# Attention and two MoE layers on one core: four raw weight buffers in the first tile, and the attention's group loop re-ordered

## The reference

```python
# attention: 8 batches x 8 heads, S = 576, D = 64, 32 memory slots
a   = softmax(phi)                          # (b, h, s, 32)
k_m = einsum('bhsm,bhsd->bhmd', a, k)       # and v_m alike
attn = softmax(q @ k_m.T / sqrt(64))        # over the 32 slots
x = (attn @ v_m)  -> (4608 tokens, 512)
# first MoE: one dense layer
h = x @ w_in                                # 512 -> 2048
x = (h * sigmoid(1.702 * h)) @ w_out        # 2048 -> 512
# second MoE: 8 experts, top 1
e = argmax(x @ w_gate); w = softmax(x @ w_gate)[e]
out = w * sigmoid(x @ w_output_gate)[e] * (relu(x @ w1[e]) @ w2[e])
```

## Time and profile before

| | us |
|---|---|
| median of 3 runs | 1346.61 (1345.87 to 1348.1) |
| the profiled execution | 1348.39 |
| its span | 1346.8 |
| PE busy | 1309.3 (97%) |
| PEld busy | 1054.9 (78%) |
| DVE busy | 634.2 (47%) |
| POOL busy | 554.6 (41%) |
| ACT busy | 388.6 (29%) |
| mean granted clock of TensorE | 0.994 |

### The profile page before, as it was taken

The page is one execution under the profiler, slowest core; times in us unless marked ns, Lnnn a source line. Parts: engine busy times, 40 slices in busy tenths (PEclk is TensorE's granted clock), DMA queues, the critical chain, the costliest instruction groups (busy, mean ns, idle before and its releaser), DMA issues.

```text
span 1346.8 us, 23538 instructions
## 1 busy us (share of the span) xinstructions
PE 1309.3 (97%) x6866; PEld 1054.9 (78%) x6867; DVE 634.2 (47%) x1291; ACT 388.6 (29%) x725; POOL 554.6 (41%) x648
## 2 busy tenths in 40 slices
PE   5997999999999999999999999999999999999997
PEld 3455888888888888888888888887788888888886
DVE  4893243443533434334334343447555555555553
ACT  3672222222222322222222222223322222222221
POOL 2455764454434442443444334512443242433332
PEclk9998999999999999999999999999999999999999
DMA  9996357555565464654654546557874778549872
GB/s 362 401 423 233 103 179 204 200 195 173 200 185 188 168 195 156 186 188 164 178 191 168 189 164 177 185 175 234 255 206 99 224 236 257 161 135 266 238 241 63
DMA packets 152924, 274.26 MB, mean 204 GB/s; under 512 B 16947, under 2 KB 54084, under 8 KB 150308
## 3 DMA queue, kind: packets, MB, share of 16 engines
q1 hardware_dynamic: 96100, 204.30, 43.6%
q10 hardware_dynamic: 43584, 37.37, 11.4%
q0 software_dynamic: 13184, 31.88, 7.4%
HBM read 144.98 MB, written 100.45 MB: 182 GB/s over the span
## 4 chain that ended last, share of the span: by engine, by line
PE 90%; DMA 4%; DVE 2%; issue 1%; POOL 1%; SPq 1%; ACT 0%; ACTq 0%; POOLq 0%
PE ps L699 29%; PE ps L733 28%; PE ps L774 15%; PE ps L803 15%; DMA phT<-in_phi 3%; PE ps L743 1%; DMA raw<-in_moe_w_out 1%; DMA raw<-in_moe_w_in 1%; DVE sc L1150 0%; DVE scs L1152 0%; DVE scs L1161 0%; PE ps L618 0%; PE ps L671 0%; POOL W L1541 0%; DMA cq<-ch 0%
## 5 line engine op out<-in xcount | busy, mean ns | idle before, releaser
L699 PE MATMUL ps<-xs,W 128*128 (+1 forms) x1728 | 420.1, 392 | 5.1 <-POOL W L1541 5.1
L733 PE MATMUL ps<-W,gs 128*128 128x512 f32 x1728 | 415.4, 389 | 1.2 <-POOL W L1531 1.1
L699 PEld LDWEIGHTS ps<-xs,W 128*128 128x128 f32 x1728 | 324.5, 189 | 75.2 <-issue 8.2
L733 PEld LDWEIGHTS ps<-W,gs 128*128 128x128 f32 x1728 | 324.5, 188 | 69.4 <-issue 1.5
L1225 DVE TENSOR_TENSOR gate<-ps,gate 128x512 f32<-128x512 f32 x144 | 99.5, 691 | 373.5 <-ACT gate L969 373.1
L969 ACT ACTIVATE gate<-ps 128x512 f32<-128x512 f32 x144 | 86.1, 598 | 474.9 <-PE ps L699 459.6
L803 PE MATMUL ps<-W,chT 128*128 (+1 forms) x936 | 218.2, 389 | 1.0 <-DVE chT L1362 0.8
L774 PE MATMUL ps<-W,cx 128*128 (+1 forms) x936 | 218.5, 389 | 0.5 <-issue 0.5
L1595 POOL CAST whi<-raw 128x512 fp32r<-128x512 f32 x128 | 83.6, 653 | 317.2 <-DMA raw<-in_moe_w 317.2
L803 PEld LDWEIGHTS ps<-W,chT 128*128 128x128 f32 x936 | 175.6, 188 | 38.1 <-issue 1.8
L774 PEld LDWEIGHTS ps<-W,cx 128*128 128x128 f32 x936 | 175.6, 188 | 37.4 <-issue 1.1
(11 more groups left out here) (163 smaller groups left out, 781.3 us busy)
## 6 DMA issues: line engine op xcount, KB each, us to landing
W<-expert_scratch SPq DMA_DIRECT2D x24, 2048.0 KB, 10.3
raw<-in_moe_w SPq DMA_DIRECT2D x128, 256.0 KB
expert_scratch<-whi SPq DMA_DIRECT2D x128, 256.0 KB, 2.6
expert_scratch<-raw SPq DMA_DIRECT2D x128, 256.0 KB, 2.8
cq<-ch ACTq DMA_DIRECT2D x156, 128.0 KB
kvm<-in_kv SPq DMA_DIRECT2D x16, 1152.0 KB, 10.6
crec<-record_scratch POOLq DMA_DIRECT2D x160, 64.0 KB
qT<-in_q SPq DMA_DIRECT2D x16, 576.0 KB, 8.6
```

The lines of the kernel that those rows point to most:

```text
L699: mm = pe.matmul(ps[:, f % 2, :], W[:, col:col + P], xs[:, bass.ds(x0 + (x_lo * K1 + c) * T, T)], start=(c == 0 and w_lo + x_lo == 0), sto ...
L733: mm = pe.matmul(ps[:, 2 + s, :], gs[:, f % 2, g_lo, s * P:(s + 1) * P], w_out_sb[:, f, w_lo, :], start=(f == 0 and g_lo + w_lo == 0), sto ...
```

## The change

Four edits.

1. Two more raw buffers (`raw2`), used in turn with the old ones from chunk 4 on; `load_w(n)` waits for the split of chunk n-4, and chunks 6 and 7 for the k/v product of group 14, since raw2 overlies kv buffer 2. Chunks 4 to 7 are issued before the store of batches 0 to 4, and the four half stores of batches 5 and 6 between the loads of chunks 8 to 11. The quarters of w_in are loaded at groups 4, 5, 9 and 10, and split by GpSimd one group later.
2. ScalarE's list: the scaled k/v product first, k's copy ahead of the exp of the scores, a's copy behind it, and the exp of phi of group g+2 (was g+1). SP loads phi two groups ahead.
3. The scores' maximum is subtracted by GpSimd (last group: by VectorE) ahead of normalize(g-2). VectorE's list is scores_max(g-1), inverses(g-2), phi's maximum of g+2, transpose of g-2. The last group's normalization has a semaphore of its own, and VectorE does both last `inverses` in a row.
4. The k/v product goes to columns 384 to 511 of bank 6, a scores' bank; it waits until VectorE has transposed that bank's half of the scores of g-1, and no longer for an output copy. mm1(0,1) stands ahead of both halves of group 14, and x_out of group 14 is between the sigmoid and the cast of step 0.

```diff
-        QUARTER = (5, 6, 9, 10)
+        QUARTER = (4, 5, 9, 10)
+        w_raw = [raw[:, 0, :], raw[:, 1, :], raw2[:, 0, :], raw2[:, 1, :]]
+        def w_slot(n):
+            return n % 2 if n < K1 else n % 4
...
             def load_w(n, src):
-                wait(sp, s_wlo, n - 1)
-                sp.dma_start(raw[:, n % 2, :], src).then_inc(s_wraw[n % 2], 16)
+                if n in (K1 + 2, K1 + 3):
+                    sp.wait_ge(s_kv, NG - 1)
+                else:
+                    wait(sp, s_wlo, n - 1 if n < K1 + 2 else n - 3)
+                sp.dma_start(w_raw[w_slot(n)], src).then_inc(s_wraw[w_slot(n)], 16)
...
-            load_kv(0)
-            load_q(0)
-            for g in range(1, NG):
-                load_phi(g)
+            load_phi(1)
+            for g in range(NG):
                 load_kv(g)
                 load_q(g)
+                if g + 2 < NG:
+                    load_phi(g + 2)
...
-            load_w(K1, w_out_v[0])
-            load_w(K1 + 1, w_in_part(0, 1))
+            for c in range(2):
+                load_w(K1 + 2 * c, w_out_v[c])
+                load_w(K1 + 2 * c + 1, w_in_part(c, 1))
             store_kept(0, FIRST, s_xfirst)
-            for b in range(FIRST, KEPT):
-                store_kept(b, 1, s_xkept)
...
-                            if f:
+                            if f >= 2:
                                 load_w(K1 + 2 * f, w_out_v[f])
+                                if f < 4:
+                                    store_kept(FIRST + f - 2, 1, s_xkept, (0,))
                                 load_w(K1 + 2 * f + 1, w_in_part(c, k))
+                                if f < 4:
+                                    store_kept(FIRST + f - 2, 1, s_xkept, (1,))
...
-                wait(pe, s_xo, 2 * (g - 4) + 1)
+                wait(pe, s_dv, DVE_A * (g - 1) + 1)
                 pe.wait_ge(s_am, g + 1)
-                out_of = lambda h: ps[h * M:(h + 1) * M, 4, 3 * P:4 * P].rearrange("p (w d) -> p w d", w=2)
+                out_of = lambda h: ps[h * M:(h + 1) * M, 6, 3 * P:4 * P].rearrange("p (w d) -> p w d", w=2)
...
             mm1(0, 0)
             out_half(NG - 3, 1)
+            mm1(0, 1)
             out_half(NG - 2, 0)
-            mm1(0, 1)
             out_half(NG - 2, 1)
...
# ScalarE
             def group(g):
                 u = g % 2
-                if g + 1 < NG:
-                    exp_phi(g + 1, 1 - u)
+                kv_scale(g, u)
                 if g >= 4:
                     x_out(g - 4, 1)
-                if g >= NG - 2:
-                    for c in range(2):
-                        first_x_hi(2 * (g - (NG - 2)) + c)
-                kv_scale(g, u)
+                if g == NG - 1:
+                    first_x_hi(2)
+                k_out(g)
                 if g:
                     exp_scores(g - 1, 1 - u)
-                k_out(g)
                 if g + 1 < NG:
                     a_out(g + 1)
+                if g + 2 < NG:
+                    exp_phi(g + 2)
+                elif g == NG - 2:
+                    first_x_hi(0)
+                    first_x_hi(1)
+                else:
+                    first_x_hi(3)
                 if g >= 3:
                     x_out(g - 3, 0)
...
# VectorE
             def group(g):
-                u = g % 2
-                if g + 1 < NG:
-                    phi_in(g + 1)
-                inverses(g, u, g >= 2, True)
-                if g:
-                    less_max(g - 1, 1 - u)
+                scores_max(g - 1, (g - 1) % 2)
+                inverses(g - 2 if g >= 2 else None, g + 1 if g + 1 < NG else None)
+                if g + 2 < NG:
+                    phi_in(g + 2)
                 if g >= 2:
                     attn_out(g - 2)
...
+            scores_max(NG - 1, 1)
+            dve.wait_ge(s_dv, DVE_A * NG)
+            dve.tensor_tensor(by_m(1), by_m(1), each_m(1, 0), ALU.subtract).then_inc(s_mx, 1)
             dve.wait_ge(b_xhi, K1)
             dve.tensor_tensor(xs[:, (2 * K1 - 1) * T:2 * K1 * T], kept(K1 - 1), xs[:, (K1 - 1) * T:K1 * T].bitcast(F32),
                               ALU.subtract).then_inc(s_x3, 1)
-            inverses(NG, 0, True, False)
-            less_max(NG - 1, 1)
+            inverses(NG - 2)
+            inverses(NG - 1)
+            dve.wait_ge(s_rin, NG + 3)
+            dve.tensor_tensor(by_m(1), by_m(1), each_m(1, 2), ALU.mult).then_inc(s_x15, 1)
             attn_out(NG - 2)
...
# GpSimd
+            def less_max(g, u):
+                pool.wait_ge(s_dv, DVE_A * (g + 1))
+                by_m = sc[u][:].rearrange("p (n m) -> p n m", m=M)
+                pool.tensor_tensor(by_m, by_m, scs[:, u, 0:1, 0:SB].rearrange("p o n -> p n o").broadcast_to([P, SB, M]),
+                                   ALU.subtract).then_inc(s_mx, 1)
             for g in range(NG):
+                if g == NG - 1:
+                    first_x_lo(0)
+                if g:
+                    less_max(g - 1, 1 - g % 2)
                 if g >= 2:
                     normalize(g - 2, g % 2)
                 v_blocks(g, g % 4)
...
-                if g == NG - 2:
-                    for c in range(2):
-                        first_x_lo(c)
+            first_x_lo(1)
             first_x_lo(2)
             normalize(NG - 2, 0)
```

More of the change, by code:

```diff
@@ L159, in build @@
             kvs = sbt(a, "kvs", [P, 2 * D])
-            kv2 = sbt(a, "kvm2", [P, QA * D * 2])
+            with ExitStack() as a2:
+                kv2 = sbt(a2, "kvm2", [P, QA * D * 2])
+            sbt(a, "before_raw2", [P, 6 * T - 2 * S - P - 2 * D])
+            raw2 = sbt(a, "raw2", [P, 2, CH])
             pT.append(sbt(a, "pT1", [P, S]))
             sbt(a, "to_512_third", [P, 64])
[L163 to L167, removed]
+            q2 = sbt(a, "qT2", [P, QA // 2, HG, M])
+            ph2 = sbt(a, "phT2", [P, S])
             qT, kvm, phT = [q0, q1, q2], [kv0, kv1, kv2], [ph0, ph1, ph2]
@@ L268, in build @@
                                                         (nc.sync, "sync_waits_passed"), (nc.tensor, "pe_waits_passed"), (nc.scalar, "act_waits_passed"))}
-        s_wraw = [sem(f"w_raw_loaded{u}") for u in range(2)]
+        s_wraw = [sem(f"w_raw_loaded{u}") for u in range(4)]
         s_whi = sem("w_hi")
@@ L452, in load_q, with store_kept @@
                 sp.dma_start(qT[g % 3][:].rearrange("p c h n -> p (c h n)"), q[g * P:(g + 1) * P, :]).then_inc(s_q[g % 3], 16)
-            def store_kept(b, n, stored):
+            def store_kept(b, n, stored, us=range(2)):
                 sp.wait_ge(s_xo, 4 * (b + n))
-                for u in range(2):
+                for u in us:
                     sp.dma_start(xT_dram[2 * u * P:(2 * u + 2) * P, b * S:(b + n) * S].rearrange("(a p) n -> p a n", a=2),
@@ L1069, in act_tile @@
                         x_hi(t + 1, f - 11)
[L1071 to L1074, removed]
+            g_sigmoid(0, 0)
+            for i in range(2):
+                x_out(NG - 2, i)
+            g_hi(0, 0)
+            for i in range(2):
+                x_out(NG - 1, i, (6, 4)[i])
             store_last()
@@ L1137, in phi_in @@
                 dve.wait_ge(s_phi[g % 3], 16 * (g // 3 + 1))
+                wait(dve, s_aT, g - 1)
                 dve.tensor_reduce(amax[:, g % 2, 0:1], phT[g % 3][:], AX.X, ALU.max, negate=True).then_inc(s_amax, 1)
@@ L1152, in less_max, with inverses, attn_out @@
                 dve.tensor_reduce(scs[:, u, 0, 0:SB], by_m(u), AX.X, ALU.max).then_inc(s_dv, 1)
[L1153 to L1160, removed]
+            def inverses(scores=None, phi=None):
+                u = scores % 2 if scores is not None else 1 - phi % 2
+                n = scores + 4 if scores is not None else phi + 1
+                lo, hi = (0 if scores is not None else SB), (SB + 1 if phi is not None else SB)
+                if scores is not None:
+                    dve.wait_ge(s_ex, scores + 1)
                     dve.tensor_reduce(scs[:, u, 1, 0:SB], by_m(u), AX.X, ALU.add).then_inc(s_sm, 1)
-                    wait(dve, s_sm, g - 1)
-                if phi:
-                    wait(dve, s_aT, g + 1)
+                    dve.wait_ge(s_sm, scores + 1)
+                if phi is not None:
+                    dve.wait_ge(s_aT, phi + 1)
                 dve.tensor_scalar(scs[:, u, 1, lo:hi], scs[:, u, 1, lo:hi], 1e-9, None, ALU.add).then_inc(s_eps, 1)
-                wait(dve, s_eps, g + 1)
+                dve.wait_ge(s_eps, n)
                 dve.reciprocal(scs[:, u, 2, lo:hi], scs[:, u, 1, lo:hi]).then_inc(s_rin, 1)
-            def attn_out(g):
-                wait(dve, s_nrm, g + 1)
+            def attn_out(g, by_pool=True):
+                if by_pool:
+                    dve.wait_ge(s_nrm, g + 1)
                 wait(dve, s_o, 2 * (g - 1))
@@ L1194, in _ @@
             phi_in(0)
+            phi_in(1)
+            dve.wait_ge(s_cst, 2 * 16)
+            inverses(phi=0)
+            inverses(phi=1)
             wait(dve, s_cst2, 6 * 16)
@@ L1206, in _ @@
```

(18 more changed lines are left out.)

60 lines of the change are left out of this document (35 added, 25 removed).

## The result

The median is 1341.43 us in 17 executions (1338.01 to 1346.16), before 1346.74 in 17 (1345.82 to 1349.06). The ratio is 0.9963, 95% interval 0.995 to 0.9975: 5.0 us faster, 3.4 to 6.7. The forecast was 6.5. The spread is the news: it has grown from 3.2 to 8.2 us, with seven executions from 1338.0 to 1340.6 (the short ones), six from 1345.7 to 1346.2 (the long ones), and only four between, among them the median. The profiled one is among the long ones: 1346.1, span 1344.5.

The account below looks back on a forecast made before the run. TensorE's matmul stream was taken to bound the kernel from its last hole, before mm1(0,4). That stream's start moves from 131.9 to 125.4 (9.3 from buffers, less the tail): 6.5 us faster, median 1340.1, range 1335.0 to 1344.5.

Parts of the forecast that it names:

- the hole in mm1(0,0): Attention's tail: TensorE idles 3.1 us before mm1(0,0)'s last quarter, waiting for GpSimd's increment of b_xlo behind normalize(14).
- the low clock behind it: Tail: the 3.1 us idle brings TensorE's lower clock, costing 2.0 us (ends 0 and 2.7) before mm1(0,2).
- Part 1: First MoE tile's weights: four buffers end the split stalls, 13.75 us from mm1(0,2) to mm1(0,4); alone worth 9.3 us.
- Part 2's loop: VectorE's attention loop per group, now 4.88 us: becomes 5.26 with eps held, 4.81 if not held.
- eps is held: VectorE's addition of eps is blocked in every group until GpSimd's new subtraction ends, 0.4 us after the sums.
- rival E: Attention loop: GpSimd's two tensor_tensors stretched from 1.16 to 1.6 us, loop 6.14; 6.3 us slower, 1352.9; chance 0.08.
- The start: Attention's first groups: phi(1) loaded first brings VectorE's first scores to 17.4 us from 20.03, 2.6 earlier.
- The step that failed: Attention on TensorE: k's copy ahead of exp and the product's wait for transposes cost nothing, covered by the output halves.
- The tail: Last scores to mm1(0,2): from 96.7 to 109.7, then 2.0 more for the clock, 111.7; what was won is given back.
- B: Clock stays up through the tail's hole (8.5 us faster), eps unheld (9.4), or both (11.4); about 1337.2; chance 0.28.
- D: TensorE's idle only moves to waits for b_xlo and kept stores, mm1(0,4) near 130; about 1346; chance 0.07.
- C: Weights stay late: chunk 11 lands 12 us after issue, mm1(0,4) at 127.4; 4.5 us faster, 1342.1; chance 0.10.

Follow-up runs that it names:

- e2: Kernel before with the four raw buffers and their load and store order alone, attention as before: median 1339.94 us, ratio 0.9944.
- e7: e5 with VectorE's inverses(g-2) ahead of scores_max(g-1) and GpSimd's normalize(g-2) ahead of the maximum's subtraction: median 1345.92 us, ratio 0.9985 to the kernel before.
- e5: Changed kernel with 8 filler matmuls ahead of the scores and 10 behind them in groups 0 to 2: median 1339.19 us, ratio 0.9938 to the kernel before.
- e9: Changed kernel with the k/v product back in bank 4, waiting for group g-4's output copy: median 1340.45 us in 5 executions, ratio 0.9945 to the kernel before.
- e12: e9's kernel run once more, product back in bank 4: median 1339.81 us in 6 executions, ratio 0.9944 to the kernel before.
- e1: Changed kernel run again without an edit: median 1339.96 us (1338.65 to 1347.07, 9 executions), ratio 0.9955 to the kernel before.
- e3: Changed kernel with two raw buffers and the old store and load order, leaving the attention's edits alone: median 1348.29 us, ratio 1.0004 to the kernel before.
- e6: e5 without the addition of 1e-9 (eps) to the attention's sums: median 1335.80 us, ratio 0.9912 to the kernel before.
- e8: e7 with GpSimd's count of x's part 3 in b_xlo ahead of normalize(14): median 1345.69 us, ratio 0.9983 to the kernel before.
- e10: e6 with GpSimd's count of x's part 3 in b_xlo ahead of normalize(14): median 1335.54 us, ratio 0.9907 to the kernel before.
- e4: Changed kernel with 32 filler matmuls ahead of the first transposes and 40 behind them: median 1343.18 us, ratio 0.9964 to the kernel before.

## Why the prediction was right, and where it was off

The sign, the range and the size (5.0 of 6.5) held, but the size by luck: two errors of opposite sign met in a median that stands between two groups of executions. mm1(0,4), forecast at 125.4 and within 123 to 126, was at 128.45 in the long execution (start +6.2, tail -3.2) and at 121.73 in the short one (-0.5 and -3.2). The last scores, forecast at 96 to 97.5, were in the range in the short one alone, and the hole in mm1(0,0) and the low clock behind it were not as forecast in either.

*Part 1* was right to 0.1 us: e2's mm1(0,4) at 122.59, predicted 122.6; 13.73 from mm1(0,2) in the changed kernel, predicted 13.75; and the splits kept 2.3 us ahead, 2.8 in e2. A split did wait for its load before mm1(0,4), 0.44 us in the long execution, 0.95 in the short one and 1.86 in e2, but none so long that TensorE had to wait.

*Part 2's loop* was right: 5.37, predicted 5.26. The lost 0.1 lies behind pT: the transposes start 0.1 after it, and take 0.85 for 0.78. That eps is held is now shown: it takes 0.57 or 0.58 in every loop from 26.29 us on, where GpSimd's subtraction stands beside it, and 0.17 or 0.18 in e7, where nothing does; without it the loop is 4.90 (4.81 predicted for the unheld one). The prediction took the hold from one row. The trace of before had a second, which also ended with a tensor_tensor of GpSimd (51.15 + 1.28 = 52.43):

```profile
51.89 0.57 DVE L1165 TENSOR_SCALAR scs<-scs 128x19 f32<-128x19 f32 x1
```

The Trainium skill's rule on the shared pair (SBUF — State Buffer, section Who interferes with whom) agrees with each of these, also in that no reduction was stretched (0.75 at most in the changed kernel, beside it as alone). The slow rival E, which needed that, didn't come, both GpSimd instructions keeping 1.16.

*The start* was right for the first scores (17.09 and 16.43, predicted 17.4), and for the last in the short execution (96.21, predicted 96.7).

*The step that failed* is the sentence that k's copy ahead of exp, and the product's wait for the transposes, "cost nothing: half of the 1.27 of two halves covers each". From group 3 on nothing is lost by them: k's copy is covered, and the up to 0.70 us for which TensorE still stands before a product are hidden by VectorE's loop of 5.37. In groups 0 to 2 there are no output halves, so TensorE stands 0.36 and 0.69 us in each, and where its clock is low everything is in series: 6.87 a loop. Filling the holes (e5) or taking the wait away (e9, e12) left no execution above 1342.3. So I had missed a term of 0 to 6.7 us that differs between executions; against e5 it is 2.3 us (e1) to 3.4 us (the 17 executions) by the ratios. I had noted the cover's price, but for loops that have it.

*The tail* was priced too high, by 3.2 us. From the last scores to mm1(0,2) I had 15.0 (109.7 - 96.7 and 2.0 for the clock); it took 11.81 and 11.78. 2.0 of that is the low clock, which didn't come: the hole in mm1(0,0) was 1.35 us, not 3.1, and the matmuls behind it kept their durations (12 in 3.04 us). 1.2 of the shorter hole is that I let the count of b_xlo wait for normalize(14)'s end: mm1(0,0) went on at 107.42, when normalize had only begun, at 107.36. The hold of the last subtraction was 0.16 us (0.92 for 0.76), not 0.7. The other steps of the tail took some 0.5 more than priced.

Of the rivals, B's first condition (the clock stays up in the tail) came true in both profiles, and the short executions have nearly its size: 1339, forecast 1337.2 to 1338.1. D and E didn't occur, nor C, since no stall on a split stands before mm1(0,4).

Open is what decides in one execution whether the clock rises at 15 or at 39 us: the two profiles have the same instructions and waits to within 0.2 us until 14.8.

## What to carry to other kernels

Before a wait is called covered, look for the iterations in which the cover isn't there yet: the first ones of a pipeline. And where TensorE has many short waits, price its loop at the low clock too; if that is longer than the bound of another engine, the time will vary from execution to execution, and a few matmuls of no use are cheap (e5). Look also for the small instruction that a move puts beside a long one: with the subtraction on GpSimd, eps grew by 0.4 us in each loop, and the re-ordered attention gained nothing that can be told (e5 against e2). And a ratio of 1.00 for half of a change says little while something else, here the weights (e3), comes last.

## What the runs showed of the hardware

- A tensor_scalar of 128 x 18 or 19 on VectorE took 0.57 to 1.29 us for 0.17 to 0.19 wherever a tensor_tensor on GpSimd ran when it came, ending with it (0.57 or 0.58 in the loops of the changed kernel, 1.29 and 1.28 once each in the kernel before and in e2). Beside such an instruction tensor_reduce kept its 0.75, reciprocal its 0.28 (e6) and the transpose to pT its 0.77 or 0.78.
- A semaphore increment by GpSimd's sequencer behind a tensor_tensor passed when this began (107.36, TensorE released at 107.42), not when it ended (108.52); e5, e6 and e7 show the same 0.06 us. So a count behind normalize costs the wait for normalize's start and not its 1.16 us. That start was late enough to leave a hole of 1.35 us in the changed kernel, 0.68 in e6 and 0.42 in e7, which went when the count stood ahead (e8, e10).
- TensorE raised to its full clock by 72 idle matmuls had it for the product at 11.22, behind a wait of 2.31 us, and no more for the transposes at 12.77. It stayed at the low level, a granted clock of 0.50, past 37 us (e4).
- Without an edit the same kernel had its full-clock durations from 14.8 us on in one execution and from some 39 us on in another. The profile's granted clock read 1.00 in this stretch of both, so a low clock at the start of a trace is to be read from durations.
